# A retention and two-mixture kernel on one core: halves of w1's odd blocks exchanged on load, rows of c stored later, division moved

## What is computed

```python
def _moe_ref(x, phi, w1, w2):
    logits = x @ phi                      # 3072 x 32
    d = exp(logits - logits.max(0)); d /= d.sum(0) + 1e-09
    slot_input = (d.T @ x).reshape(E, S_per_e, D)     # 8 experts, 4 slots each, 512
    for e in range(E):
        h = np.maximum(slot_input[e] @ w1[e], 0.0)    # w1[e]: 512 x 1024
        slot_out[e] = h @ w2[e]                       # w2[e]: 1024 x 512
    c = exp(logits - logits.max(1)); c /= c.sum(1) + 1e-09
    return c @ slot_out
```

## Time and profile before

| | |
|---|---|
| median of 3 runs | 378.9 us (378.09 to 380.42) |
| profiled execution | 380.2 us, span 378.3 us |
| PE, DVE, ACT, POOL busy | 337.1, 142.8, 133.6, 106.8 us |
| moved by DMA | 67.39 MB |

### The profile page before, as it was taken

How to read it: one execution, slowest core, us unless ns; L and a number is a source line. 1 busy time by engine, 2 the same in 40 slices (tenths; PEclk the granted TensorE clock), 3 DMA queues, 4 the chain that set the end, 5 groups by cost and what they waited for, 6 DMA issues and landing times.

```text
span 378.3 us, 8140 instructions
## 1 busy us (share of the span) xinstructions
PE 337.1 (89%) x3138; PEld 253.9 (67%) x3139; DVE 142.8 (38%) x262; ACT 133.6 (35%) x240; POOL 106.8 (28%) x111
## 2 busy tenths in 40 slices
PE   6899999999999997999660879999999999999990
PEld 4788778776887864233150358888888888888870
DVE  2665546455545444412028994312220222202200
ACT  6445544453553532012000263514432243423300
POOL 4212212122122200005000145545444545444231
PEclk9999999999999998899965569999999999999997
DMA  9999989999999999699804700221111111111010
GB/s 219 249 283 308 268 221 294 265 305 265 264 298 281 273 342 385 218 381 389 312 2 158 289 29 19 68 71 54 58 58 42 69 42 63 55 52 56 31 61 30
DMA packets 81963, 67.39 MB, mean 178 GB/s; under 512 B 52648, under 2 KB 65144, under 8 KB 81920
## 3 DMA queue, kind: packets, MB, share of 16 engines
q1 hardware_dynamic: 77808, 57.25, 52.0%
q0 software_dynamic: 4096, 9.53, 7.1%
q10 hardware_dynamic: 16, 0.02, 0.0%
HBM read 58.91 MB, written 7.88 MB: 177 GB/s over the span
## 4 chain that ended last, share of the span: by engine, by line
PE 62%; SPq 16%; DMA 13%; DVE 3%; issue 2%; POOL 1%; ACT 1%; POOLq 0%; DVEq 0%
PE ps L1437 32%; SPq L301 7%; DMA W<-in_moe_w_dram 6%; SPq L289 5%; DMA W<-in_k_dram 5%; PE psAB L1291 4%; PE ps L1514 3%; PE psAB L1428 3%; PE psAB L1225 3%; PE psAB L1199 3%; DMA W<-in_q_dram 2%; SPq L345 2%; PE ps L1217 2%; PE psAB L1232 2%; PE ps L1146 1%
## 5 line engine op out<-in xcount | busy, mean ns | idle before, releaser
L1021 DVE SCALAR_TENSOR_TENSOR h_low<-psAB,h_high 128x1024 fp32r<-128x1024 f32 x24 | 28.3, 1219 | 99.1 <-ACT h_high L554 99.1
L643 POOL TENSOR_TENSOR W<-W,cst 128x512 f32<-128x512 f32 x24 | 25.8, 1073 | 101.9 <-DMA W<-in_k_dram 87.6
L566 ACT ACTIVATE yout<-ps,gates 128x512 f32<-128x512 f32 x24 | 16.5, 689 | 87.6 <-PE ps L1437 86.3
L1437 PE MATMUL ps<-w_high,h_high 128*128 x176 | 44.6, 395 | 0.0
L1437 PE MATMUL ps<-w_low,h_high 128*128 x176 | 43.5, 389 | 0.0
L1437 PE MATMUL ps<-w_high,h_low 128*128 x176 | 43.5, 389 | 0.0
L676 POOL DMA_INDIRECT out_dram<-yout,target x24 | 24.2, 1010 | 62.0 <-ACT yout L566 61.3
L797 DVE TENSOR_TENSOR W<-psAB,cst 128x1024 f32<-128x1024 f32 x24 | 29.4, 1223 | 24.2 <-PE psAB L1199 24.1
L1437 PEld LDWEIGHTS ps<-w_low,h_high 128*128 128x128 f32 x176 | 33.0, 188 | 7.0
L1437 PEld LDWEIGHTS ps<-w_high,h_low 128*128 128x128 f32 x176 | 33.0, 188 | 6.9
L670 POOL DMA_INDIRECT part<-token_rows,token x24 | 23.2, 966 | 50.1 <-DVE token L977 38.0
(11 more groups left out here) (241 smaller groups left out, 458.9 us busy)
## 6 DMA issues: line engine op xcount, KB each, us to landing
W<-in_moe_w_dram SPq DMA_DIRECT2D x36, 512.0 KB, 6.8
W<-in_moe_w_dram SPq DMA_DIRECT2D x7, 2048.0 KB, 11.1
W<-in_q_dram SPq DMA_DIRECT2D x12, 512.0 KB, 6.8
W<-in_k_dram SPq DMA_DIRECT2D x24, 256.0 KB, 5.9
W<-in_v_dram SPq DMA_DIRECT2D x24, 256.0 KB, 6.9
W<-in_moe_w_dram SPq DMA_DIRECT2D x2, 1024.0 KB, 6.1
w_raw<-in_moe_w_dram SPq DMA_DIRECT2D x4, 512.0 KB, 9.1
token_rows<-rows POOLq DMA_DIRECT2D x4, 384.0 KB, 7.9
```

What stands on the lines that cost most here:

```text
L643: nc.gpsimd.tensor_tensor(ks[n % 2].rearrange("p (h d) -> p h d", h=H), k_raw[n % 3].rearrange("p (h d) -> p h d", h=H), fac, ALU.mult).th ...
L1021: V.scalar_tensor_tensor(h_low[u][:, part_of], psAB[:, part_of], 0.0, h_high[u][:, part_of].bitcast(fp32), ALU.max, ALU.subtract).then_inc ...
L1437: return mm(z, of_tile(h, v)[:, j, :], w[:, ds(at + j * DM, DM)], **flags)
```

## The change

It has these parts:

1. **Loads of w1's odd blocks.** `quarter_w1` issues two loads of 64 partitions (256 KB each) instead of one of 128, with the halves exchanged. There are 16 odd blocks, so SP issues 16 loads more; the bytes stay the same. `first_layer` waits for 6 loads instead of 4.
2. **Join of the products.** x's odd blocks stay exchanged, and the slots come from 4 products of 128 columns instead of 2 of 128 and 4 of 64.
3. **Division moved.** `seln` is the selection times `last_shrink` alone, made right behind `lead_exp`. The product for the sum (`den_ready`) stands behind the slot products on PE, DVE makes `inv` after the own slots, and ACT multiplies with it when it copies h.
4. **Last copy of x divided.** In the last chunk ACT copies one PSUM bank of y and DVE the other, at the same time. DVE's work on the last but one group moves from the start of the last chunk to behind the loop.
5. **Rows of c stored later.** POOL waits for the last quarter of w2[7] before it issues the four stores to `token_rows`.

```diff
             def quarter_w1(e, slot, at):
-                sp.dma_start(W[:, slot * SLOT + at * F:slot * SLOT + (at + 1) * F], w1[e, at * P:(at + 1) * P, :]
-                             ).then_inc(w_in[slot], 16)
+                to, rows_of = W[:, slot * SLOT + at * F:slot * SLOT + (at + 1) * F], w1[e, at * P:(at + 1) * P, :]
+                if at % 2 == 0:
+                    sp.dma_start(to, rows_of).then_inc(w_in[slot], 16)
+                    return
+
+                for side in range(2):
+                    sp.dma_start(to[side * D:(side + 1) * D, :], rows_of[(1 - side) * D:(2 - side) * D, :]
+                                 ).then_inc(w_in[slot], 16)
...
-                nc.scalar.activation(xT[n % 2].rearrange("p (jj o) t -> p o jj t", o=2),
-                                     y_banks.rearrange("p o (jj t) -> p o jj t", t=P), ACT.Copy).then_inc(xT_copied, 1)
+                own = slice(0, 2 if n + 1 < NT else 1)
+                nc.scalar.activation(xT[n % 2].rearrange("p (jj o) t -> p o jj t", o=2)[:, own],
+                                     y_banks.rearrange("p o (jj t) -> p o jj t", t=P)[:, own], ACT.Copy
+                                     ).then_inc(xT_copied, 1)
...
-                nc.scalar.activation(yout[f][:, :], psA[:, f * 512:(f + 1) * 512], ACT.Copy
+                if f == 0:
+                    act.wait_ge(inv_ready, 1)
+                nc.scalar.activation(yout[f][:, :], psA[:, f * 512:(f + 1) * 512], ACT.Copy, scale=inv[:, 1:2]
                                      ).then_inc(h_copied, 1)
...
             pool.wait_ge(rows_built, 1)
+            pool.wait_ge(last_in[QUARTERS - 1], 16)
...
-                if n >= GROUP + 3 and n % GROUP == 3:
+                if n >= GROUP + 3 and n % GROUP == 3 and n < NT - 1:
                     sum_group(n // GROUP - 1)
                     add_group(n // GROUP - 1)
...
+            sum_group(last_group - 1)
+            add_group(last_group - 1)
+            dve.wait_ge(y_ready, NT + 3)
+            V.tensor_copy(xT[(NT - 1) % 2].rearrange("p (jj o) t -> p o jj t", o=2)[:, 1],
+                          y_banks.rearrange("p o (jj t) -> p o jj t", t=P)[:, 1]).then_inc(xT_copied, 1)
             max_group(last_group)
...
             dve.wait_ge(lead_exp, 1)
+            V.tensor_scalar(seln[:, :], sel, last_shrink, None, ALU.mult).then_inc(seln_ready, 1)
             V.tensor_tensor(lead_sum, last_shrink, col_sum, ALU.mult).then_inc(lead_sum_ready, 1)
             add_group(last_group)
-            dve.wait_ge(den_ready, 1)
-            done(V.tensor_scalar(inv[:, 0:1], psU[:, 260:261], 1e-9, None, ALU.add))
-            done(V.reciprocal(inv[:, 1:2], inv[:, 0:1]))
-            done(V.tensor_tensor(col_inv, inv[:, 1:2], last_shrink, ALU.mult))
-            V.tensor_scalar(seln[:, :], sel, col_inv, None, ALU.mult).then_inc(seln_ready, 1)
...
+            dve.wait_ge(den_ready, 1)
+            done(V.tensor_scalar(inv[:, 0:1], psK[:, P:P + 1], 1e-9, None, ALU.add))
+            V.reciprocal(inv[:, 1:2], inv[:, 0:1]).then_inc(inv_ready, 1)
             row_shift()
...
-            pe.wait_ge(lead_sum_ready, 1)
-            mm(psU[:, 260:261], const("rep"), lead_sum, start=True, stop=True).then_inc(den_ready, 1)
             pe.wait_ge(seln_ready, 1)
             pe.wait_ge(group_added, NT // GROUP)
             for j in range(KD):
-                if j % 2 == 0:
-                    mm(psU[:, j * SL:(j + 1) * SL], part[:, j * P:(j + 1) * P], seln[:, :], start=True, stop=True)
-                    continue
-                for side in range(2):
-                    half = j * P + (1 - side) * D
-                    last = mm(psU[side * D:(side + 1) * D, j * SL:(j + 1) * SL], part[:, half:half + D], seln[:, :],
-                              start=True, stop=True)
+                last = mm(psU[:, j * SL:(j + 1) * SL], part[:, j * P:(j + 1) * P], seln[:, :], start=True, stop=True)
             last.then_inc(slotT_ready, 1)
+            pe.wait_ge(lead_sum_ready, 1)
+            mm(psK[:, P:P + 1], const("rep"), lead_sum, start=True, stop=True).then_inc(den_ready, 1)
```

More of the change, by code:

```diff
@@ L47 @@
 QUARTERS = 4
+LOADS_W1 = QUARTERS + 2
 def retention_two_mixtures(nc, q, k, v, phi, w1, w2, emb, tau, w1b, w2b, consts, out):
@@ L230, in retention_two_mixtures @@
         rmax_ready, row_shifted, row_exp = sem("rmax_ready"), sem("row_shifted"), sem("row_exp")
-        h_half = sem("h_half")
+        h_half, inv_ready = sem("h_half"), sem("inv_ready")
         seln_ready, slotT_ready, slotT_copied = sem("seln_ready"), sem("slotT_ready"), sem("slotT_copied")
@@ L1149, in logits_T @@
             def logits_T(n):
-                pe.wait_ge(xT_copied, n + 1)
+                pe.wait_ge(xT_copied, n + 1 if n + 1 < NT else NT + 1)
                 for j in range(KD):
@@ L1179, in sum_x @@
                 pe.wait_ge(x_kept, GROUP * (g + 1) + 1)
+                if g:
+                    pe.wait_ge(group_added, g)
                 for r in range(GROUP):
@@ L1276, in _ @@
             for j in range(KD):
-                if j % 2 == 0:
-                    mm(psU[:, j * SL:(j + 1) * SL], part[:, j * P:(j + 1) * P], seln[:, :], start=True, stop=True)
-                    continue
-                for side in range(2):
-                    half = j * P + (1 - side) * D
-                    last = mm(psU[side * D:(side + 1) * D, j * SL:(j + 1) * SL], part[:, half:half + D], seln[:, :],
-                              start=True, stop=True)
+                last = mm(psU[:, j * SL:(j + 1) * SL], part[:, j * P:(j + 1) * P], seln[:, :], start=True, stop=True)
             last.then_inc(slotT_ready, 1)
+            pe.wait_ge(lead_sum_ready, 1)
+            mm(psK[:, P:P + 1], const("rep"), lead_sum, start=True, stop=True).then_inc(den_ready, 1)
             def first_layer(e):
                 pe.wait_ge(slotT_copied, e + 1)
-                pe.wait_ge(w_in[e], 16 * QUARTERS)
+                pe.wait_ge(w_in[e], 16 * LOADS_W1)
                 for f in range(2):
@@ L1300, in second_layer @@
                 if e < E - 1:
-                    pe.wait_ge(w_in[slot], 16 if e < 3 else 16 * (QUARTERS + 1))
+                    pe.wait_ge(w_in[slot], 16 if e < 3 else 16 * (LOADS_W1 + 1))
                 pe.wait_ge(hT_copied, e + 1)
```

## The result

The changed kernel took 392.21 us in the median of 4 runs (387.29 to 395.05), the kernel before 378.5 us in the median of 4 (375.65 to 380.42). The ratio is 1.0357, with a 95% interval of 1.0285 to 1.0429: 13.5 us slower, where 2.2 us faster was forecast, and outside the stated range of 372.5 to 386.5 us. The likeliest case was wrong. Rival B, the halves at half rate and in step, holds the result between its two sums: 387.5 us if gaps absorb 7.8 us, 395.3 us if they absorb nothing.

A forecast was written before the change was run, and what follows sets the result against it. Attention was taken as held by PE and DMA nearly in balance, the mixture by PE's tail, then DMA. Stores -4.0, tail -1.2 and halves +3.0 gave -2.2 us, from 378.9 to 376.7 us, range 372.5 to 386.5.

The forecast's parts named there:

- The likeliest case: Whole kernel: the forecast of 376.7 us with all terms as priced, 374.5 to 380 us, chance 0.38.
- Rival B: w1's loads in attention: halves go at half rate, in step; 387.5 us, or 395.3 without absorption; chance 0.22.
- nearly in balance: Attention, 20 to 130 us: PE busy 106.69 of 110 us and DMA's share 1.03, both holding it.
- The end of the loop: Last y ready at 141.4 us: unmoved if halves are free, 144.4 as forecast, 150 or more for rival B.
- Stores later: Second layer: moving 1.57 MB of stores behind the last quarter frees DMA for weights, 4.0 us gained (3 to 4.5).
- rival C: Second layer: stores move but weights don't use the 4 us, as loads wait for `h_ready`; 380.7 us, chance 0.10.
- Tail: Attention's end to first layer: earlier products 0.73, join 0.3, divided copy 0.2, together 1.2 us gained (0.3 to 1.9).
- SP's 16 issues: Attention: 16 more issues, 6.9 us of SP's time, priced at nothing because SP stands before a full queue.
- I take half, 0.68 us a block: w1's halved loads: 0.68 us more a block, between nothing and 1.35; 10.8 us for 16 blocks.
- they don't run in step: DMA engines in attention: share swings from 0.88 to 1.10 among stretches, so they aren't all on the same half together.
- The estimate of 1.07 us a block: w1's halved loads by the Trainium skill's rates: 1.07 us more a block, 17 us in all, about 383 us total.
- of the 10.8 us the gaps absorb the 7.8 us: Attention's DMA: best stretch 297 GB/s, mean 276, so 7% of 110 us are gaps; 3.0 us remain as lengthening.

The follow-up runs named there:

- e7_stores: The kernel before with one part alone, the stores of c's rows waiting for the last weight quarter: 373.59 us, ratio 0.9922.
- e8_tail: The kernel before with only the division moved and the last copy of x divided, six slot products: 375.34 us, ratio 0.9966.
- e1_whole: The changed kernel with w1's odd blocks in one load each and six slot products, the other parts kept: 372.29 us, ratio 0.9864 to the kernel before.
- e10_uneven: The kernel before with each of w1's 16 odd blocks in two 128-partition loads of 992 and 32 columns: 378.26 us, ratio 1.0015.
- e9_w2_halves: The kernel before with w2[3] to w2[6] each loaded by two loads of 64 partitions: 392.38 us, ratio 1.0418.
- e2_halves: The kernel before with each of w1's 16 odd blocks in two loads of 64 partitions, not exchanged: 396.11 us, ratio 1.0495.
- e12_two_queues: As e9_w2_halves, but POOL issues the upper halves, so both lie ready in two queues: 384.91 us, ratio 1.0213 to the kernel before.
- e15_eight_blocks: The kernel before with one block of each expert's w1, 8 in all, in two loads of 64 partitions: 386.77 us, ratio 1.0237.

## Why the prediction was wrong, point by point

**The bound.** Right for the mixture: PE's tail, and then DMA. For attention, "nearly in balance" was half right: DMA had no reserve at all (see the absorption). The end of the loop was named as the place that decides, and it moved from 141.4 to 155.6 us, with attention at 245 GB/s, as rival B was to show itself.

**Stores later.** Forecast 4.0 us (3 to 4.5). Behind SP's last issue the trace of the changed kernel has 4.1 us less and that of e7_stores 4.0; in time e7_stores gave 2.9 us (1.8 to 4.1), just under the lower bound. The mechanism was right, the size about so; rival C is out.

**Tail.** Forecast 1.2 us (0.3 to 1.9), of it 0.3 from the join. The trace shows 1.7, of which about 0.7 is a higher clock, and e8_tail, without the join, 1.3 us (0.2 to 2.3). So 0.2 us for the copy, 0.6 for `seln` and 0.2 for the join are left, 1.0 in all, within the bounds. The clock was taken as between its two levels during the products; it was at 0.50 before and at 1.00 after (1.00 in e1_whole's trace too, 0.50 in e8_tail's), so that part of the trace's 1.7 is luck.

**SP's 16 issues.** Priced at nothing: e10_uneven, 0.6 us with no change inside its interval. Right.

**The halves' price.** Here the prediction fell. The step "I take half, 0.68 us a block" had 1.35 us as its upper bound; it is 1.0 us in the stretch that DMA alone bounds (e9_w2_halves) and 1.2 in attention (e2_halves). The reason given was that a half rate needs all engines on one half at once and that "they don't run in step". The conclusion was wrong: 211 to 231 GB/s against 386 is not far above half. The first part may hold, since e12_two_queues with both halves in flight was faster. The swing of DMA's share among stretches of 10 us says nothing about whether engines are in step over the 1.35 us of a block. For this, the Trainium skill had the better figure. "SBUF — State Buffer", "Door 1: The DMA port swizzle", gives about 218 GB/s as the limit of partitions 0 to 63, and the windows of e9_w2_halves agree within 6% (211 to 231). The estimate of 1.07 us a block from its rates at 1 MiB, set beside rival B, is what the runs show within 10% (1.0 and 1.2). The same page of the Trainium skill, in its section "Can I just issue two DMAs to hit both halves?", says that two concurrent loads at partitions 0 and 64 give only 6% more than one. In e12_two_queues, with two queues, they gave 310 GB/s against 220, 40% more; the measurement decides.

**The absorption.** The step "of the 10.8 us the gaps absorb the 7.8 us" fell entirely: e15_eight_blocks added 9.0 us where all was to be absorbed. The 7% between the best and the mean stretch weren't room. A stretch can be slow because of what it moves, and PE, itself busy for 106.7 of 110 us, can't make up for a load that is late. Which of the two it was, is argued and not shown. Part of the 7% was also a trait of the one trace it was read from: e7_stores, whose loads in attention are the same, moved 284 GB/s in that stretch, and the 276 of the kernel before are the lowest of the untouched ones.

**The sum anew.** With the measured terms: halves +18.7, stores -2.9, tail -1.3, join -0.2 make +14.3; measured was 13.5 (10.8 to 16.2). The chances were the other error. Rival B had a row-based upper bound and a page for it, the forecast only a guess at half, and B got 0.22.

## What to carry to other kernels

Don't split a load into halves of the partitions in a stretch where DMA is full: a 512 KB block cost 1.0 to 1.2 us more, and what it bought on PE was 0.2 us. In this kernel, with DMA's share about 1 and SP waiting to issue, the first 16 blocks turned every added microsecond of DMA into at least one of time; slower stretches were no reserve. Stores that nobody reads soon belong behind the last load that someone waits for.

## What the runs showed of the hardware that I had not expected

- Loads to one half of the partitions, one half after the other in one queue: 211 to 231 GB/s, against 356 to 405 for the same bytes over 128. Even partitions, then odd ones: only 4.0 us for 16 blocks instead of 18.7.
- The two halves side by side in two queues: about 310 GB/s, 205 of them in POOL's queue and 107 in SP's. The queues got through equally many packets (317 and 315 in 6 us), POOL's of 3.9 KB and SP's of 2.0 KB; full-width loads in the same two queues were divided the same way (402 and 405).
- Stores beside halves: 376 GB/s together, where the halves alone had 211 to 231.
- Cutting 4 KB rows into 2 KB ones, to all partitions, cost 3.7 to 6.2 us for 16 blocks inside attention, while 992 + 32 columns cost 0.6.
- Halves issued by POOL beside SP's loads in attention made it worse than from SP alone: 230 GB/s against 245, with k's loads landing after 7.4 us instead of 5.9.
